# Rotary embedding in an attention and MLP kernel: a small table for the first pair, raw data double-buffered, high parts by GpSimd, stacks made in the round of their scores

## What is computed

```python
def rotate(x):
    x1, x2 = (x[..., :half], x[..., half:])
    return np.concatenate([x1 * cos - x2 * sin, x1 * sin + x2 * cos], axis=-1)
q_rot, k_rot = (rotate(q), rotate(k))
scores = np.matmul(q_rot, k_rot.transpose(0, 1, 3, 2)) / np.sqrt(64)
attn = softmax(scores)                       # by row, less the row's maximum
x = matmul(attn, v), heads joined            # 4 x 576 x 512
x = x + relu(layernorm(x, g_ln) @ w_ch1) @ w_ch2
h = gelu(x @ w_in); u, v = halves of h
out = x + (u * (w_sg @ layernorm(v) + b_sg)) @ w_out
```

## Time and profile before

| | us |
|---|---|
| median of 3 runs | 966.39 (965.19 to 966.91) |
| profiled execution, its own time | 961.98 |
| its span | 960.2 |
| PE busy | 920.8 |
| DVE busy | 526.2 |
| ACT busy | 399.8 |
| POOL busy | 221.5 |
| mean granted TensorE clock | 0.998 |

### The profile page before, as it was taken

The page is one execution under the profiler, slowest core; times in us unless marked ns, Lnnn a source line. Parts: engine busy times, 40 slices in busy tenths (PEclk is TensorE's granted clock), DMA queues, the critical chain, the costliest instruction groups (busy, mean ns, idle before and its releaser), DMA issues.

```text
span 960.2 us, 15722 instructions
## 1 busy us (share of the span) xinstructions
PE 920.8 (96%) x5577; PEld 822.5 (86%) x5577; DVE 526.2 (55%) x926; ACT 399.8 (42%) x858; POOL 221.5 (23%) x213
## 2 busy tenths in 40 slices
PE   1799999999999699999999999999999999999998
PEld 1699999999999688889888888888888998989897
DVE  3699999999999744323221132123224664563624
ACT  1799999999998333211210110112123231302111
POOL 4876776776741000000000000000000100010100
PEclk9999999999999999999999999999999999999999
DMA  4333233233321233210000000001200001000011
GB/s 129 96 95 84 77 93 83 75 93 84 77 53 29 82 100 106 66 44 1 1 1 1 1 0 0 0 0 62 83 12 1 1 1 44 1 32 24 1 44 55
DMA packets 44822, 43.99 MB, mean 46 GB/s; under 512 B 14112, under 2 KB 34720, under 8 KB 44640
## 3 DMA queue, kind: packets, MB, share of 16 engines
q1 hardware_dynamic: 44768, 43.26, 16.1%
HBM read 28.56 MB, written 4.72 MB: 35 GB/s over the span
## 4 chain that ended last, share of the span: by engine, by line
PE 92%; DVE 4%; issue 1%; POOL 1%; ACT 1%; DMA 1%; SPq 0%; POOLq 0%; DVEq 0%; ACTq 0%
PE hid_ps L1544 21%; PE acc_ps L1558 20%; PE ring_ps L1454 9%; PE scores_ps L1390 6%; PE wide_ps L1668 6%; PE ring_ps L1401 6%; PE wide_ps L1650 5%; PE bank_ps L1682 5%; PE bank_ps L1630 5%; PE scores_ps L1383 2%; PE ring_ps L1340 2%; DVE nmax L1021 1%; DVE prob_lo L1030 1%; PE ring_ps L1412 1%; PE ring_ps L1422 1%
## 5 line engine op out<-in xcount | busy, mean ns | idle before, releaser
L1544 PE MATMUL hid_ps<-xT,W1s 128*128 128x512 f32 (+1 forms) x960 | 211.6, 370 | 4.6 <-DVE xT L1098 4.6
L1558 PE MATMUL acc_ps<-W2s,hid 128*128 128x512 f32 x864 | 210.5, 391 | 0.0
L1544 PEld LDWEIGHTS hid_ps<-xT,W1s 128*128 128x128 f32 x960 | 169.7, 189 | 36.9 <-DVE xT L1098 4.6
L1183 DVE SCALAR_TENSOR_TENSOR hid<-hid_ps,hid 128x512 fp32r<-128x512 f32 (+1 forms) x80 | 51.0, 637 | 253.9 <-ACT hid L886 253.9
L1558 PEld LDWEIGHTS acc_ps<-W2s,hid 128*128 128x128 f32 x864 | 160.5, 188 | 32.6 <-DVE hid L1183 0.2
L886 ACT ACTIVATE hid<-hid_ps 128x512 fp32r<-128x512 f32 (+1 forms) x80 | 44.4, 555 | 305.2 <-PE hid_ps L1544 305.2
L1021 DVE TENSOR_REDUCE nmax<-scores_ps 128x1 f32<-128x576 f32 x144 | 106.7, 748 | 13.6 <-PE scores_ps L1390 11.7
L807 ACT ACTIVATE E<-scores_ps,nmax 128x576 f32<-128x576 f32 x128 | 96.2, 752 | 5.5 <-DVE nmax L1021 4.7
L1030 DVE TENSOR_TENSOR prob_lo<-ring_ps,prob_hi 128x512 fp32r<-128x512 f32 x144 | 95.2, 678 | 0.8 <-ACT prob_hi L821 0.7
L821 ACT ACTIVATE prob_hi<-ring_ps 128x512 fp32r<-128x512 f32 x144 | 83.3, 606 | 8.0 <-PE ring_ps L1401 6.5
L763 POOL TENSOR_TENSOR rstd<-ve,power 128x1 f32<-128x1 f32 x18 | 14.6, 813 | 306.1 <-DVE ve L1254 306.1
(11 more groups left out here) (135 smaller groups left out, 1447.4 us busy)
## 6 DMA issues: line engine op xcount, KB each, us to landing
swapped_k<-stack SPq DMA_DIRECT2D x64, 144.0 KB, 2.4
w_raw<-in_w SPq DMA_DIRECT2D x32, 256.0 KB, 3.1
qk_raw<-in_q SPq DMA_DIRECT2D x16, 256.0 KB, 2.8
qk_raw<-in_k SPq DMA_DIRECT2D x16, 256.0 KB, 2.6
v_raw<-in_v SPq DMA_DIRECT2D x16, 256.0 KB, 2.6
out<-out_sb SPq DMA_DIRECT2D x14, 256.0 KB, 2.2
w_raw<-in_win SPq DMA_DIRECT2D x4, 512.0 KB, 4.2
rotary<-rotary_table SPq DMA_DIRECT2D x2, 576.0 KB, 4.2
```

The source lines that it names most:

```text
L1183: nc.vector.scalar_tensor_tensor(out=hid[:, f % 2, 1, 0:cols], in0=hid_ps[:, f % 2, 0:cols], scalar=0.0, in1=hid[:, f % 2, 0, 0:cols].bitc ...
L1544: mm = nc.tensor.matmul(hid_ps[:, f % 2, 0:cols], W1s[:, slot1(f), w, c, :], xT[:, x, c, 0:cols], start=first, stop=(c == DC - 1 and x == 1))
L1558: mm = nc.tensor.matmul(acc_ps[:, t, :], hid[:, f % 2, x, P * t:P * t + P], W2s[:, slot2(f), w, :], start=(f == 0 and x == 0 and w == 0), ...
```

## The change

- rotary_tables also gives a first table for pair 0, 240 KB: cosines for the five tiles of head 0 and the tails, and sines of half the width. Its tiles are in the order of the slots: four of head 0, the tails, four of head 1; so are all q and k tiles now.
- Pair 0 is roped by DVE alone (first_rope), first the five tiles of slots 0 to 4 and then the other four, k before q, with scalar_tensor_tensor, whose scalar brings the factor 1/8 or the sign. The high parts of the first five tiles are made by ACT (first_high), the rest by DVE. PE's first stacks wait for each half by itself. q of pair 0 is loaded from ACT's queue. ACT also rounds ident_r.
- qk_raw has room for two pairs. q and k of pair 1 are loaded at the start, between the two large tables, and those of pair r + 2 wait for the rope of pair r.
- From pair 1 on POOL makes the high part itself, by a second add into qk_split; DVE's casts are gone from the rounds.
- The stacks of pair r (TL, Q0, Q1, K1) are made in round r, that of K0 at the end of the round before.
- The order of all bodies and the ring are new. DVE's and SP's steps lie one round nearer to the scores (rounds from -2 instead of -3).

The diff, cut to its core:

```diff
@@ waits and loads
+        def raw_tiles(p, which):
+            at = (2 * p.odd + which) * NQK * D
+            return qk_raw[:, at:at + TILES * D].rearrange("p (t d) -> p t d", d=D)
...
@@ block.sync
-            sp.dma_start(rotary[:, 0].rearrange("p a t d -> p (a t d)"), table_dram[:, 0]).then_inc(table_in[0], 16)
-            load(sp, pair(0), 0)
-            sp.dma_start(rotary[:, 1].rearrange("p a t d -> p (a t d)"), table_dram[:, 1]).then_inc(table_in[1], 16)
+            sp.dma_start(first_rotary, first_dram).then_inc(first_table_in, 16)
             load(sp, pair(0), 1)
-            sp.dma_start(ident[:, :], eye_dram).then_inc(const_in, 16)
+            sp.dma_start(ident[:, :], eye_dram).then_inc(ident_in, 16)
+            for which in range(2):
+                sp.dma_start(rotary[:, which].rearrange("p a t d -> p (a t d)"), table_dram[:, which]).then_inc(table_in[which], 16)
+                load(sp, pair(1), which)
+            sp.wait_ge(zeroed, 1)
+            load_v(sp, pair(0))
...
             def body(r):
                 load_qk(r + 2, 1)
-                swap_keys(r, 0)
+                load_values(r)
+                swap_keys(r, 1)
+                keep_o(r - 2, 0)
                 load_qk(r + 2, 0)
-                keep_o(r - 3, 0)
-                keep_o(r - 3, 1)
-                swap_keys(r, 1)
-                load_values(r)
+                keep_o(r - 2, 1)
+                swap_keys(r + 1, 0)
...
@@ block.gpsimd
+            def qk_high(p, which):
+                if not live(p) or is_round(p, 0):
+                    return
+                pool.wait_ge(rope_step, last_of(rope_order, p, [(step, which) for step in ("scale", "cross0", "cross1")], 1))
+                wait_filled(pool, p - 1, ("QK"[which], 0), ("QK"[which], 1), ("TL", 0))
+                nc.gpsimd.tensor_tensor(qk_split[:, which, :, 0:D], rot[:, which], cross[:, which], ALU.add).then_inc(split_hi[which], 1)
...
             def body(r):
+                scale(r + 1, 1)
+                v_low(r - 1)
+                crosses(r + 1, 1, 1)
                 crosses(r + 1, 1, 0)
-                scale(r + 1, 1)
+                crosses(r + 1, 0, 0)
                 scale(r + 1, 0)
-                crosses(r + 1, 0, 0)
+                crosses(r + 1, 0, 1)
+                qk_high(r + 1, 1)
+                qk_high(r + 1, 0)
+                add(r + 1, 1)
                 add(r + 1, 0)
-                keep_rinv(r - 3)
-                add(r + 1, 1)
+                qk_low(r + 1, 1)
                 qk_low(r + 1, 0)
-                qk_low(r + 1, 1)
-                v_low(r - 1)
-                crosses(r + 2, 1, 1)
-                crosses(r + 2, 0, 1)
+                keep_rinv(r - 1)
...
@@ block.scalar
+            load(act, pair(0), 0)
+            act.wait_ge(ident_in, 16)
+            nc.scalar.activation(ident_r[:, :], ident[:, :], ACT.Copy).then_inc(ident_ready, 1)
+            first_high(1)
+            first_high(0)
             def body(r):
+                exp(r - 1, 5)
+                copy_o(r - 2, 1, 1)
+                prob_high(r - 1, "QT", 0)
+                copy_stack(r, 0, 1)
                 copy_stack_tails(r)
...
@@ block.vector
             def first_rope():
...
+                own, other = slice(0, NT + 1), slice(NT + 1, NQK)
+                dve.wait_ge(first_table_in, 16)
+                dve.wait_ge(qk_in[0][1], 48)
+                first_products(1, own)
+                dve.wait_ge(first_rot, 3)
+                first_add(1, own)
+                dve.wait_ge(qk_in[0][0], 48)
+                first_products(0, own)
+                dve.wait_ge(first_rot, 7)
+                first_add(0, own)
+                dve.wait_ge(first_hi, 1)
+                first_low(0, 1, own)
+                first_products(1, other)
+                dve.wait_ge(first_hi, 2)
+                first_low(0, 0, own)
...
             def body(r):
...
-                if not is_round(r + 1, 0):
-                    qk_high(r + 1, 0)
...
@@ block.tensor, the new body
+                make_stack_tails(r)
+                score(r - 1, 7)
+                transpose_group(r - 1, 0, 3)
+                times_v(r - 2, 1, 0, all)
+                make_stack(r, 0, 0)
+                score(r - 1, 8)
+                make_stack(r, 1, 0)
+                transpose_group(r - 1, 1, 0)
+                transpose_o(r - 2)
+                transpose_group(r - 1, 0, 1)
+                score(r, 0)
+                make_stack(r, 1, 1)
+                transpose_key_tails(r - 1)
+                score(r, 1)
...
+                transpose_query_tails(r)
+                score(r, 6)
+                make_stack(r + 1, 0, 1)
```

More of the change, by code:

```diff
@@ L29, in rotary_tables @@
     tail = seq - full * 128
[L30 to L37 removed]
+    first = np.zeros((128, 2, full + 1, half), np.float32)
+    for n, row in enumerate((cos, sin)):
+        first[:, n, :full] = row[: full * 128].reshape(128, full, half)
+        for h in range(2):
+            first[h * tail:(h + 1) * tail, n, full] = row[full * 128:]
+    tiles = list(range(full + 1)) + list(range(full))
+    cosines = np.concatenate([first[:, 0], first[:, 0]], 2)[:, tiles]
+    sines = np.concatenate([-first[:, 1], first[:, 1]], 2)[:, tiles]
+    table = np.stack([cosines, sines], 1)
+    first = np.concatenate([cosines[:, :full + 1].reshape(128, -1), first[:, 1].reshape(128, -1)], 1)
+    return first, np.stack([table * np.float32(scale), table], 1)
 @dataclass(frozen=True)
@@ L867, in _ @@
+                exp(r, 4)
+                copy_o(r - 1, 0, 0)
+                prob_high(r, "G0", 0)
+            rounds(act, body, (-2, 0))
             act.wait_ge(scores, PAIRS * NQK)
@@ new lines, in first_cross @@
+            def first_cross(which, tiles, a):
+                factor = (0.125 if which == 0 else 1.0) * (2 * a - 1)
+                n = tiles.stop - tiles.start
+                c = cross[:, which, tiles, :].rearrange("p t (a d) -> p t a d", a=2)
+                nc.vector.scalar_tensor_tensor(out=c[:, :, a], in0=raw_halves(pair(0), which, tiles)[:, :, 1 - a], scalar=factor,
+                                               in1=first_sin[:, 0:n], op0=ALU.mult, op1=ALU.mult).then_inc(first_rot, 1)
@@ new lines, in first_add, with first_low, first_products @@
+            def first_add(which, tiles):
+                nc.vector.tensor_tensor(rot[:, which, tiles], rot[:, which, tiles], cross[:, which, tiles], ALU.add).then_inc(first_rot, 1)
+            def first_low(h, which, tiles):
+                nc.vector.tensor_tensor(qk_split[:, which, tiles, D:2 * D], rot[:, which, tiles],
+                                        qk_split[:, which, tiles, 0:D].bitcast(f32), ALU.subtract).then_inc(first_lo[h][which], 1)
+            def first_products(which, tiles):
+                first_scale(which, tiles)
+                for a in range(2):
+                    first_cross(which, tiles, a)
@@ L1352, in make_stack_tails @@
                     mm = nc.tensor.transpose(bank("TL", 0)[:, P * which:P * which + P].bitcast(f32r),
[L1353 removed]
+                                             qk_split[:, which, NT, :], ident_r[:, :])
                 mm.then_inc(filled, 1)
```

394 lines of the change are left out of this document (181 added, 213 removed), and 18 rows, old and new, of tables (RING_JOBS, filled_order).

## The result

| | us |
|---|---|
| before, median of 4 runs beside it | 965.79 (964.04 to 966.91) |
| after, median of 4 runs | 949.18 (948.01 to 949.96) |
| ratio | 0.983, 95% interval 0.981 to 0.985 |
| profiled execution of after, its own time | 949.65, span 947.8 |
| forecast | 945.3 (938.5 to 954.0) |

The change makes the kernel 16.6 us faster. The forecast was 21.1; sign and range were right, and 4.5 us of the gain did not come. Four later sets of runs of the kernel before have medians of 964.0 to 964.8; against those the gain is 14.9 to 15.7 us, still well inside the interval.

The account below looks back on a forecast made before the run. PE (17.1 us) and DVE (17.3) stood close under the 18.0 us round, neither alone the bound. First MLP matmul at 47.0 + 13 x 17.6 + 14.8 + 20.5 = 311.1, 21.1 earlier: 966.4 - 21.1 = 945.3 us, range 938.5 to 954.

Parts of the forecast that it names:

- The round: Attention loop, one pair of heads per round: from 18.0 to 17.6 us, 5.3 us over 13 rounds, ends 0 and 11.7.
- PE's sum: PE's work per attention round, estimated from matmul and transpose starts: 17.1 us, unchanged and becoming the largest term.
- The tail score's 1.4: Term of PE's round: eight matmuls, four of 512 and four of 64 columns, put at 1.4 us by rate per column.
- Rival 2: Attention rounds: PE runs at its sum, 17.1 us a round; 27.8 us gained, 938.6 us; chance 0.15.
- Rival 1: Attention rounds: stay at 18.0 us, swap chain or POOL's port replacing DVE; 15.5 us gained, 950.9; chance 0.25.
- The first pair: Start of the kernel: first maximum of pair 0 at about 15.6 us instead of 29.10.
- Pair 1: Start: POOL's rope done at 25.9 us, first maximum at 31.5 instead of 43.43.
- Pair 2: Start: POOL again, 15.7 us with v_low; first maximum at 47.0 instead of 60.85, 13.9 us gained, ends 11 and 16.
- The end: Pair 15 through to the first MLP matmul: 14.8 us instead of 15.2, then 20.5 instead of 22.0.
- the drain: Last maximum to first MLP matmul: 1.5 us off 22.0, ends 0 and 3.
- the 4.4 us: Profiled execution before (961.98 us) lay 4.4 under the 966.39 median; forecast taken from the median, 966.4 - 21.1.
- Rival 4: Start: data or port hold POOL, so pair 2 gains 7 us instead of 13.9, rounds 17.6; 952.2; chance 0.08.

Follow-up runs that it names:

- e1: Kernel after, but POOL adds in place and DVE casts the high parts of q and k from pair 1 on, as before; 951.46 us.
- e4: Kernel after without the swapped-key products in score slots 2 and 7, 0.53 us less PE work per pair; 945.8 us.
- e9: Kernel after with the cast of v's high part moved from ACT to DVE; 968.89 us, ratio 1.004.
- e12: Kernel after with the cast of v on DVE instead of ACT, as two casts of five tiles instead of one of ten; 955.36 us.
- e6: Kernel after with DVE's four normalising operations of the first MLP block spread over round 16, behind the last maximum; 945.95 us.
- e5: Kernel before, unchanged, run again for a second profile; median 964.43 us, profiled execution 965.14 us.
- e2: Kernel after with pair 0 roped from the two whole 576 KB tables instead of the small first table; 950.33 us.
- e8: Kernel after with 24 more transposes ahead of the first MLP matmul to keep PE busy; 949.51 us.
- e11: Kernel after with normalising spread over the last round and the first two blocks of MLP weights loaded in SP's round 15; 943.35 us, ratio 0.978.
- e3: Kernel after with q and k of pair r + 2 loaded only once POOL has roped pair r + 1, as with a single raw buffer; 950.47 us.
- e7: Kernel after with 28 idle PE matmuls of 512 columns in the first 14 us; 948.8 us.
- e10: Kernel after with PE holding pair 0's third score until POOL has made k's low part of pair 1; 957.19 us.

## Why the prediction was right, and where it was off

**The round: right in size, half right in cause.** The forecast was 17.6, picked between the bounds 17.1 and 18.0, so that the exact hit is part luck. Measured are 17.6 in eight rounds and 17.67 on average over all 13, 4.5 us instead of 5.3. DVE came to 16.2 (16.0), POOL to 16.0 (15.8), POOL's wait went where it was put. But I gave the gain to the casts, and e1 gives them 0.15 of 0.4 in the steady rounds and 0.19 of 0.35 over all 13; the rest is left for the new order, which I priced at nothing. PE's sum is not firm either. The tail score's 1.4 does not follow from the rate per column, which gives 8 x 0.13 = 1.0, though the trace before has 1.36 for it. Summed over eight rounds, the median distance from each line's matmuls to the next gives 17.4 us a round before and 17.3 after, but the median for each pair of neighbours 16.8 and 16.6: estimates that bracket the 17.1 and don't settle it. Rival 2 (the round falls to 17.1) did not come; e4 shows that the floor under 17.6 is not PE's alone.

**The port.** Rival 1 (the round stays at 18.0), by the sentence of the Trainium skill's "Perfetto Trace Analysis", section "Optimizing Scalar/DVE Operations", fell for the casts: e1 to after, moving them from DVE to POOL gained 2.3 us (2.4 in the 13 rounds of the traces). But the port itself is real here, in two places. At the start it cost 1.2 us (12.75, above). And e9, which moved a cast from ACT to DVE, lost 19.7 us: 13.5 of them by the port, since e12 gets these back by the shape of the cast alone, and 6.2 by the work that DVE has more.

**The first pair: right within 0.7.** 16.3 against 15.6, by another path than the one that I summed. I had the swapped keys land last, at 14.6 to 16.7. They are in time: PE goes from the last stack, at 14.41, to the scores without a wait, and that stack waited for DVE's last step, which POOL held up by 1.2 us at 12.75. The text named this, with 13.7, without taking it; it measured 14.4.

**Pair 1: off by 2.0.** 33.5 against 31.5. POOL was done at 26.9, not 25.9, since it started 1.0 later, at 12.68 behind DVE. The other 1.0 lies between it and the maximum, 6.6 us instead of 5.6. I had put the end of PE's round 0 at 25.4, just ahead of POOL. At half clock until 26 us, which I had not priced, it ended at 27.4, and the first stack of pair 1 then stood 0.39 us behind DVE's prob_lo for its bank:

```profile
27.92 0.51 PE L1388 MATMUL ring_ps<-ident_r,qk_split 128*128 128x128 f32 x4 [0.39 <-DVE prob_lo L1080]
```

From there to the maximum it is 5.6 us, as priced.

**Pair 2: off by 4.5 in all, the step that failed.** "POOL again, 15.7 us with v_low". The first maxima of pairs 1 and 2 are 18.0 us apart. POOL was in time: its last step of pair 2 ends at 42.6 and PE makes the first stack of it at 45.22, 2.6 us later. What lies between the two maxima is a full round of PE, DVE and ACT, which I had counted everywhere but here:

```profile
39.78 2.80 POOL L730 TENSOR_TENSOR qk_split<-rot,qk_split 128x576 fp32r<-128x576 f32 x2
...
45.22 0.45 PE L1388 MATMUL ring_ps<-ident_r,qk_split 128*128 128x128 f32 x4
```

```profile
33.50:51.50 18.00, 17.86 (x145) 17.51 (x146) 16.35 (x28) 17.12 (x41) 16.65 (x15) 1.00 0.37 90
```

The right way to price a fill is the largest of all chains for each step: for pair 1 POOL's, for pair 2 the round's. The step from 31.5 to 47.0 was 15.5 us (my terms, 41.6 and 5.6 behind it, would have given 47.2); with 18.0 in its place the forecast would have had 2.5 us of the 4.5, and pair 1 has the other 2.0.

**The end: off by 3.1.** I took 0.4 off pair 15 and 1.5 off the drain, with bounds of 0 and 3; they came out 0.8 and 0.4 longer. The bounds left out a loss, and the prediction gives no reason for that. For the drain the place is shown by e6: `normalise(0)` stands ahead of the Y that PE waits for (2.71 us), and putting it elsewhere gives 3.2 us in the median. Pair 15 is as long in e6 as in after (16.0), so its 0.8 us has another cause. In that stretch PE waits 1.1 us for DVE's prob_lo, the longer time (0.67) right behind statistics of the MLP that DVE does at 295.4, where before it had no such wait; no run tests this.

**From the trace to the median: 4.8 us the other way.** The terms above are 8.5 us short (319.6 against 311.1; the MLPs add 0.2), but the median is only 3.9 over the forecast. I had carried over the 4.4 us by which the profiled execution before lay under its median. After's own lies 0.5 over its median. e5 shows why: the profile I read was of an execution that lost little clock in its drain, and most lose more. Against e5's trace the gain is 963.4 - 947.8 = 15.6 us in spans, near the 16.6 of the medians; there the fill is 9.4 of it, and the drain is 22.4 against 24.3 us. How much of these 1.9 us is clock isn't parted: both have a stretch of 3.4 us at half clock in it, and e5 another 2.0 us before the first MLP matmul. That a profiled execution lies 0.5% under its median is a finding to explain before forecasting, not an offset to keep.

**Rival 4** (the start doesn't do it, 952.2) was half the truth: pair 2 gained 9.3, between its 7 and my 13.9, though not for its reason (neither data nor port held POOL up by more than 1 us).

## What to carry to other kernels

Price a pipeline's first rounds like the others: the largest of all engines' chains, not the one that the change is about. When the order of a tuned loop changes, look at the one-off work hung on its last rounds: 2.5 us of DVE work ahead of one release cost 3.2, and moving it and four loads to other places gave 5.8. Before an element-wise copy is put beside a busy GpSimd, look at what its shape does to the port: its time alone says nothing.

## What was not expected of the hardware

**One cast waits for GpSimd and another doesn't, by shape.** Nine or five tiles of 64 into rows of a larger buffer: 0.73 and 0.48 us, beside POOL as elsewhere. Ten tiles: 0.48 alone, 1.6 in the median beside POOL. And four tiles, at the start of after:

```profile
11.56 0.28 DVE L1057 CAST qk_split<-rot 128x256 fp32r<-128x256 f32 x1
```

From 0.48 for 320 elements and 0.73 for 576, 256 elements would take 0.41 us (an estimate). They take 0.28: this even one is faster than the odd ones, as the ten tiles are (0.48, where the same line gives 0.80). POOL was idle then, so it shows the rate and not a wait.

The Trainium skill has both halves of it, on two pages. "SBUF — State Buffer", section "SBUF: two separate sides", says that a DVE operation in a two-port mode holds the pair of ports that GpSimd uses for the whole instruction, and the other way round. "Vector Engine (DVE) Microarchitecture Reference", section "Performance modes — why throughput varies by op and dtype", says that a copy between places in SBUF takes that mode if the outermost dimension of input and output can be split alike, that is even, or odd and equal. An input that is one run of 576 or 320 elements and an output of 9 or 5 rows fail it; 640 and 10 pass, and so do 256 and 4. The traces agree: e12's 474 to 485 ns against e9's 481 to 7045. The tensor_scalar of 9 elements in, 9 out passes too, and is the one that waits (0.15 at its shortest, 0.9 in the mean of eight rounds in after).

**An idle time of PE of about 3 us is followed by half its clock in one execution and not in another.** Ten of the kernels from after on have the same idle time of 2.7 us in the drain. Nine of their traces show 1.2 GHz for 3.4 us from its end or just behind it; e2's has 2.4 GHz throughout (columns as in the earlier trace rows):

```profile
303.70:307.70 4.00, 3.75 (x31) 3.54 (x30) 3.14 (x7) 2.60 (x6) 0.00 (x0) 1.00 0.01 4
```

Before the first MLP matmul ten of these traces have an idle time of 2.9 to 3.6 us; e8 and e11 have 0.4 and 0.5. The stretch of half clock there, and the time from that matmul to the end:

| half clock | traces | to the end, us |
|---|---|---|
| none | e2 (idle 3.3), e4 (3.1), e8, e11 | 626.6 to 626.7 |
| 3.4 us | after, e3, e6, e12 (idle 2.9 to 3.6) | 628.2 to 628.3 |
| 6.8 us | e1, e7, e9, e10 (idle 2.9 to 3.6) | 629.3 to 629.6 |

So the length of the idle time doesn't tell which it will be, and one such stretch costs 1.5 us. A shorter one can do it too: e7's fall at 26.0 stands behind 1.4 us. On the whole the times of one kernel go with its mean clock: e3's four runs took 947.7 us at a mean clock of 1.000, 950.1 and 950.9 at 0.995 and 0.996, and 952.1 at 0.993. e11, whose runs have 0.998 to 1.000, spreads over 0.4 us, after and e8 over 2.0 and 3.0. It isn't all: e8 took 947.6 us at 0.996 and 948.6 at 0.998. What the clock has of the spread was not tried by itself.
